# Two-phase fp32 kernel on one core: new order of the seven-product sums, an earlier split of w_out2, and GpSimd for the operands' low parts

## What is computed

```python
# attention part, batch 8, 8 heads, S = 576, head size 64
kv  = einsum('bhsd,bhse->bhde', k, v)
out = einsum('bhsd,bhde->bhse', q, kv)
x   = out / sqrt(mean(out**2) + 1e-6) * g_norm          # -> (8, 576, 512)
# first MLP
h = relu(x @ w_in); u, v = h[..., :512], h[..., 512:]
v_n = (v - mean(v)) / sqrt(var(v) + 1e-6)
x = (u * (w_spatial @ v_n + b_spatial)) @ w_out
# second MLP
h = relu(x @ w_in2)                                      # 512 -> 1024
conv = 3-tap convolution of h along S, one set of taps per feature
out = (h * sigmoid(conv)) @ w_out2                       # 1024 -> 512
```

## Time and profile before

| | us |
|---|---|
| median of 3 runs | 841.52 (839.79 to 842.79) |
| the profiled execution's own time | 841.8 |
| its span, first to last instruction | 840.0 |
| PE busy | 802.4 (96%) |
| DVE busy | 607.5 (72%) |
| ACT busy | 418.3 (50%) |
| POOL busy | 41.1 (5%) |

### The profile page before, as it was taken

One profiled execution on the slowest core, in us unless ns is written; L12 is line 12 of the kernel. 1 busy time (PEld: TensorE's weight loads), 2 busy tenths in 40 slices (PEclk: granted clock), 3 DMA queues, 4 the chain that ended last, 5 costly groups with the idle time before them and its releaser, 6 DMA issues.

```text
span 840.0 us, 16008 instructions
## 1 busy us (share of the span) xinstructions
PE 802.4 (96%) x5910; PEld 704.0 (84%) x5910; DVE 607.5 (72%) x1254; ACT 418.3 (50%) x753; POOL 41.1 (5%) x44
## 2 busy tenths in 40 slices
PE   8998999999999999999969999999999999999998
PEld 7678899897979899898868897978879797796976
DVE  3876666757665766758869878597885978669782
ACT  4654352526343443524715648456473655646563
POOL 3342000000000000000140000000000000000000
PEclk9999999999999999999979999999999999999999
DMA  9862433426262533331322111121201212102101
GB/s 317 276 238 58 181 115 120 179 75 248 71 253 57 197 105 116 106 92 64 114 85 99 51 35 65 64 99 51 99 22 42 98 50 98 50 13 98 50 1 62
DMA packets 34009, 88.48 MB, mean 105 GB/s; under 512 B 2514, under 2 KB 8882, under 8 KB 30004
## 3 DMA queue, kind: packets, MB, share of 16 engines
q1 hardware_dynamic: 33828, 87.99, 31.0%
q10 hardware_dynamic: 144, 0.01, 0.0%
HBM read 61.92 MB, written 26.08 MB: 105 GB/s over the span
## 4 chain that ended last, share of the span: by engine, by line
PE 71%; DVE 18%; ACT 4%; issue 4%; DMA 2%; SPq 0%; DVEq 0%; ACTq 0%
PE ps L446 23%; PE ps L622 17%; PE ps L614 14%; PE ps L477 11%; DVE h_and_sums L1172 3%; DVE work L1213 3%; DVE work L1208 3%; PE ps L397 2%; DVE v_hg_split L1219 2%; PE ps L413 2%; ACT v_hg_split L897 2%; DMA kv_raw<-kv_rest_dram 1%; PE ps L547 1%; DVE t_then_s L1092 1%; PE ps L425 1%
## 5 line engine op out<-in xcount | busy, mean ns | idle before, releaser
L622 PE MATMUL ps<-w_in_split,v_hg_split 128*128 128x512 f32 x832 | 209.1, 398 | 14.7 <-DVE v_hg_split L1219 13.9
L622 PEld LDWEIGHTS ps<-w_in_split,v_hg_split 128*128 128x128 f32 x832 | 151.8, 188 | 66.0 <-DVE v_hg_split L1219 33.5
L446 PE MATMUL ps<-w_sp_split,v_hg_split 128*128 128x288 f32 x896 | 122.2, 297 | 2.8 <-DVE w_sp_split L1061 2.4
L446 PEld LDWEIGHTS ps<-w_sp_split,v_hg_split 128*128 128x128 f32 x896 | 120.8, 190 | 3.5 <-issue 2.6
L446 PE MATMUL ps<-x_operand_split,w_in_split 128*128 128x288 f32 x768 | 104.3, 296 | 1.5 <-ACT work L704 1.5
L446 PEld LDWEIGHTS ps<-x_operand_split,w_in_split 128*128 128x128 f32 x768 | 102.2, 188 | 3.6 <-ACT work L704 1.9
L477 PE MATMUL ps<-w_in_split,x_operand_split 128*128 128x512 f32 x384 | 93.5, 396 | 0.0
L477 PEld LDWEIGHTS ps<-w_in_split,x_operand_split 128*128 128x128 f32 x384 | 70.4, 188 | 20.9 <-issue 6.1
L1172 DVE TENSOR_TENSOR h_and_sums<-t_then_s,ps 128x288 f32<-128x288 f32 x64 | 28.0, 453 | 62.0 <-PE ps L614 41.5
L1172 DVE TENSOR_TENSOR h_and_sums<-h_and_sums,ps 128x288 f32<-128x288 f32 x160 | 66.2, 449 | 8.2 <-PE ps L614 7.4
L614 PE MATMUL ps<-x_operand_split,w_combined_more 128*128 128x288 f32 x384 | 62.3, 298 | 0.0
(11 more groups left out here) (124 smaller groups left out, 1137.4 us busy)
## 6 DMA issues: line engine op xcount, KB each, us to landing
kv_raw<-kv_main_dram SPq DMA_DIRECT2D x8, 2048.0 KB, 9.7
q_raw<-q_T_dram SPq DMA_DIRECT2D x8, 1152.0 KB, 5.3
operand_scratch<-t_then_s SPq DMA_DIRECT2D x8, 1152.0 KB, 5.3
operand_raw<-operand_scratch SPq DMA_DIRECT2D x8, 1152.0 KB, 5.5
out_dram<-work SPq DMA_DIRECT2D x32, 256.0 KB, 2.2
sq_then_r<-r_scratch SPq DMA_DIRECT2D x14, 576.0 KB, 6.3
operand_scratch<-work SPq DMA_DIRECT2D x24, 288.0 KB, 2.6
operand_more_raw<-operand_scratch SPq DMA_DIRECT2D x8, 864.0 KB, 7.2
```

Source lines behind the costliest of these rows:

```text
L446: last = pe.matmul(pair[bank][:, c, :], st, mo[:, c * HALF:(c + 1) * HALF], start=(n == 0), stop=(n == len(steps) - 1))
L622: last = pe.matmul(PS[:, ROW_BANK[i], :], x, wout2[:, w, F_ORDER[e], :], start=(e == 0 and n == 0), stop=(e == FT - 1 and n == len(PASSES) ...
```

## The change

1. The seven products come in the order A11, S2, A12, S1, S4, S3, A22, and the sums of a group follow in the order u2, C11, u4, C12, u3, C22, C21 (before: u2, C11, u3, u4, C22, C21, C12). The upper feature block of a group is complete after sum 4, the lower after sum 7, and `F_ORDER` takes them in turn.
2. The queues of `body2` on ACT and DVE are written out by hand instead of by a loop over e. `h_lo(0)` and `h_lo(1)` stand within the sums of groups 2 and 3.
3. For the batches ahead, `operand_lo` moves from DVE to POOL, and ACT makes three of the seven high parts ahead of its last two `h_hi`.
4. w_out2 is loaded in two halves by DMAs in ACT's queue in batches 1 and 2 of the first phase, split there by ACT (four instructions a batch) and POOL, sent to a scratch in HBM (2 MB each half), and loaded back split (four DMAs, 4.2 MB in all) ahead of the second phase.
5. `square_sum` contracts all 128 partitions: 16 matmuls for 32 before, and the inverse root works on 144 columns for 288.
6. For the last batch the T blocks are made within the sums of the second phase's first group. The waits on the stores move from the head of the second phase to the first `sigmoid` and the first copy out. A12 and A22 get other places for their high parts, with one wait less.

The core of the diff:

```diff
-PRODUCTS = [(A11, B11), (S2, T2), (A12, B21), (S3, T3), (S1, T1), (A22, T4), (S4, B22)]
+PRODUCTS = [(A11, B11), (S2, T2), (A12, B21), (S1, T1), (S4, B22), (S3, T3), (A22, T4)]
-LAST_SUM = [None, 0, 1, 2, 4, 5, 6]
-F_ORDER = [4, 0, 5, 1, 6, 2, 7, 3]
-TOP_SUM, LOW_SUM = 6, 5
+LAST_SUM = [None, 1, 2, 6, 4, 5, 7]
+F_ORDER = [0, 4, 1, 5, 2, 6, 3, 7]
+TOP_SUM, LOW_SUM = 4, 7
...
+            def operand_lo(b, k):
+                o = PRODUCTS[k][1]
+                pool.wait_ge(s_ophi, b * NPROD + k + 1)
+                pool.tensor_tensor(operand[o][:, LO, :], operand_raw[o], operand[o][:, HI, :].bitcast(F32),
+                                   ALU.subtract).then_inc(s_oplo, 1)
...
+                    if isinstance(b, int) and b in (1, 2):
+                        if i == 0:
+                            wo2_load(b - 1)
+                        else:
+                            wo2_split(b - 1, i - 1)
...
+            def wo2_split(h, f):
+                act.wait_ge(s_wo2_in, (h + 1) * DMA)
+                act.activation(wo2_hi[:, f, :], wo2_raw[:, f, :], ACT.Copy).then_inc(s_wo2_hi, 1)
...
-                for e in range(FT + 2):
-                    if e < FT:
-                        h_relu(b, e)
-                        tap1(b, e)
-                    if e >= 2:
-                        h_hi(b, odd, e - 2)
-                    if 0 <= e - 1 < FT:
-                        sigmoid(b, e - 1)
-                    if e + 1 < GROUPS:
-                        first_copy(b, e + 1)
+                h_relu(b, 1)
+                first_copy(b, 1)
+                tap1(b, 1)
+                sigmoid(b, 0)
+                h_relu(b, 2)
+                sigmoid(b, 1)
+
+                tap1(b, 2)
+                first_copy(b, 2)
+                h_hi(b, odd, 0)
+                h_relu(b, 3)
+                tap1(b, 3)
+                sigmoid(b, 2)
+                h_relu(b, 4)
+
+                first_copy(b, 3)
...
+                h_hi(b, odd, 5)
+                sigmoid(b, 7)
+                if ahead:
+                    operand_hi(b + 1, 0)
+                    operand_hi(b + 1, 1)
+                h_hi(b, odd, 6)
+                if ahead:
+                    operand_hi(b + 1, 2)
+                h_hi(b, odd, 7)
```

More of the change, by code:

```diff
@@ L151, in build @@
         u2, u3, u4 = (HB[:, o + i * HALF:o + (i + 1) * HALF] for i in range(3))
[L152 to L155, removed]
+        t_sb = [WK[:, 0:S], WK[:, 3840:3840 + S]]
+        x1 = [WK[:, S:S + HALF], WK[:, 3328:3328 + HALF]]
+        p_sb = [WK[:, 1024 + i * S:1024 + (i + 1) * S] for i in (0, 1)]
         def gated(k, l):
@@ L1221, in body2 @@
             def body2(b, odd, ahead):
-                sums_a(b, 0)
-                sums_b(b, 0)
-                sums_c(b, 0)
-                for e in range(FT + 2):
-                    g = e + 1
-                    if g < GROUPS:
-                        sums_a(b, g)
-                    if e < FT:
-                        tap0(b, e)
-                    if g < GROUPS:
-                        sums_b(b, g)
-                    if e >= 2:
-                        h_lo(b, odd, e - 2)
-                    if e < FT:
-                        tap2(b, e)
-                    if g < GROUPS:
-                        sums_c(b, g)
-                    if 0 <= e - 1 < FT:
-                        mul(b, e - 1)
@@ L1241, in body2 @@
-                if ahead:
-                    for k in range(NPROD):
-                        operand_lo(b + 1, k)
+                first = isinstance(b, int) and b == 0
+                sum_u2_c11(b, 0)
+                if first:
+                    t_a(B - 1)
+                sum_u4(b, 0)
+                sum_c12(b, 0)
+                if first:
+                    t_b(B - 1)
+                sum_u3(b, 0)
+                if first:
+                    t_c(B - 1)
+                sum_c22(b, 0)
@@ new lines, in body2 @@
+                sum_c21(b, 0)
+                sum_u2_c11(b, 1)
+                tap0(b, 0)
+                sum_u4(b, 1)
+                tap2(b, 0)
+                sum_c12(b, 1)
+                sum_u3(b, 1)
+                tap0(b, 1)
+                sum_c22(b, 1)
+                sum_c21(b, 1)
+                tap2(b, 1)
+                sum_u2_c11(b, 2)
+                mul(b, 0)
+                sum_u4(b, 2)
+                tap0(b, 2)
+                sum_c12(b, 2)
+                sum_u3(b, 2)
@@ new lines, in body2 @@
+                h_lo(b, odd, 0)
+                sum_c22(b, 2)
+                sum_c21(b, 2)
+                tap2(b, 2)
+                sum_u2_c11(b, 3)
+                mul(b, 1)
+                sum_u4(b, 3)
+                tap0(b, 3)
+                sum_c12(b, 3)
+                sum_u3(b, 3)
+                h_lo(b, odd, 1)
+                sum_c22(b, 3)
+                sum_c21(b, 3)
+                tap2(b, 3)
+                mul(b, 2)
+                for e in range(4, FT):
+                    tap0(b, e)
+                    h_lo(b, odd, e - 2)
+                    tap2(b, e)
+                    mul(b, e - 1)
@@ L1245, in _ @@
+                h_lo(b, odd, FT - 2)
+                mul(b, FT - 1)
+                h_lo(b, odd, FT - 1)
             for i in range(FT):
```

196 lines of the change are left out of this document (124 added, 72 removed).

## The result

| | before | after |
|---|---|---|
| median, us | 841.39 (839.79 to 842.79) | 874.88 (872.61 to 875.95) |
| span of the profiled execution | 840.0 | 872.1 |
| second phase begins | 416.84 | 433.11 |
| batches 0, 1, 2, 3 of the second phase | 60.82, 53.70, 47.74, 53.82 | 52.93, 57.12, 52.24, 57.29 |
| mean granted TensorE clock | 0.992 | 0.982 |

The change makes the kernel slower: ratio 1.0395, 95% interval 1.0365 to 1.0425. The direction was forecast, the size was not: +33.5 us where +15.3 was forecast, and 874.9 lies above the range. The 32.1 us of span fall into two halves of like size: 16.3 in the first phase (forecast +6.4), 15.8 in the second (forecast +8.9). Of the 16.3, 2.4 us are a start-up that came later in this execution, which differs from run to run.

A forecast was written before the change was run, and what follows sets the result against it. It took second-phase row steps to be bound by the ACT-DVE chain, 2.98 us against the PE's 2.73. Terms 6.4 - 8.0 + 16.9 = +15.3 gave 856.8 us; range 838 to 863 for 8 in 10.

The forecast's parts named there:

- beside the other I take 6 (bounds 4 and 8): First phase, batches 1 and 2: w_out2's load beside the kv load lands in 6 us; +3.2 us a batch.
- The sum: Whole kernel: first phase +6.4, second phase's batch 0 -8.0, its batches 1 to 7 +16.9, together +15.3 us.
- the forecast wait on the squares: First phase, batches 1 and 2: fourth square starts at 18.5 instead of 15.6, so the PE waits 1.3 us.
- the exclusion: Second phase, batch end: DVE and POOL lock each other out of one port pair; even batch 50.5, without it 49.25.
- The walk: Each engine's fixed queue followed forward with traced durations; gave +2.9 us for an even second-phase batch, +2.6 for an odd one.
- The price from the earlier trace: DVE subtractions beside POOL take 1.77 us against 0.75 alone; DVE waits 1.25 us for a 576-column POOL instruction.
- a lag of 2.4: Second phase, batch 0: T blocks and pad memsets put DVE's seventh sum 2.4 us late, a lag that stays.
- the tail: Second phase, batch end: early high parts and POOL delay the last `h_lo` to 47.7 us from 44.4; batch ends at 50.5.
- The openings of groups 2 and 3: Second phase: ACT's opening copies stand behind sigmoids, so DVE idles about 1.9 us per group.
- Rival 2: Second phase: group openings not late, `h_lo(2)` done at 27.9 us, row steps closed but for the tail; 823 us, chance 0.15.
- Rival 1: Second phase: POOL barely hinders DVE; even batches 49.25, odd 55.15 us, total 846 us, chance 0.17.
- rival 3: Gains and losses cancel: load lands in 4 us, `square_sum` gains 4, POOL costs half; 842.5 us, chance 0.10.

The follow-up runs named there:

- the larger pieces: Changed kernel with w_out2's rows dealt so each partition reads one 8 KB piece instead of four of 2 KB (output of permuted rows): 866.85 us.
- C and D undone: Changed kernel with all seven high parts back behind the last `h_hi` and the low parts back on DVE: 848.32 us.
- the three ways of A: Changed kernel with w_out2's splits behind u's relus, or its load one batch earlier, or its load in 8 KB pieces: 855.51, 856.62, 866.85 us.
- B: Changed kernel with the first copies of groups 2 and 3 moved ahead of the sigmoids in ACT's queue: 846.01 us.
- A, B and C with D: Changed kernel with w_out2's splits behind u's relus, first copies early, high parts late, low parts on DVE; all together: 803.00 us.

## Why the prediction was wrong

**The step that failed first: "beside the other I take 6 (bounds 4 and 8)".** The load of w_out2 landed in 14.2 and 10.1 us. The sum had the kv load running from 2.5 us into the batch. SP's timelines have it issued at 5.0 before the change (238.44, the batch begins at 233.40) and at 5.1 in batch 1 after it, and the q load at 13.6 in both. So kv was still on its way when w_out2's load was issued, 8.3 us in, and q, which the sum left out, came before it had landed. Issued ahead of the others it does land in 6.5 us (load one batch earlier): 6 was the price of another place in the program. A better upper bound is an estimate from all bytes in flight: kv's 2304 KB, q's 1152 and the load's 1024 are 4.6 MB, at the 331 GB/s of the window after the change 13.9 us. That it comes so near to 14.2 is in part luck: some of kv had been moved by 100.20, and a store of 1152 KB issued at 95.99 was still on its way.

**What the wait costs a second time.** Neither PE wait was forecast above 2 us, and the clock not at all; the forecast wait on the squares did not come. In a batch without a wait, the matmuls of the rest and the sum of squares take 3.0 us from the start of one to the end of the other (219.34 to 222.36). Behind the wait of 7.32 us in batch 1 they take 5.5, behind the 3.15 us of batch 2 5.9, and with the larger pieces 5.5 behind 3.83 us and 4.7 behind 2.54. So the lower clock cost 2.5, 2.9, 2.5 and 1.7 us there: much the same behind 3.2 us as behind 7.3. In all, batches 1 and 2 cost 10.6 + 6.5 = 17.1 where 6.4 was taken: 10.5 of waiting, 5.4 of clock, and the rest for the splits and what follows from them (0.6 a batch in the load-early kernel).

**What the first phase gave back** was missed: its batch 0 takes 49.4 us for 52.1. The sum said that the PE doesn't wait for DVE in the first phase, which is true of steady batches only: in batch 0 the PE's wait for the spatial weights' low parts fell from 2.41 us to 1.27, and the spatial products behind it take 15.08 us for 16.61 (15.01 in a steady batch). In the profile of after this is hidden by the start-up that came 2.4 us later (the second kv product starts at 38.8 to 42.5 us in the profiles here). The row of before:

```profile
75.66 16.61 PE L446 MATMUL ps<-w_sp_split,v_hg_split 128*128 128x288 f32 x112 [2.41 <-DVE w_sp_split L1061]
```

That the shorter inverse root is what frees it was not tried by itself. `square_sum` takes 1.19 us for 1.24: worth nothing, as taken.

**POOL beside DVE: right mechanism, a term too small.** The sum gave the exclusion 1.25 us in an even batch (50.5 against 49.25) and 1.2 in an odd one. Undoing it gave 2.9 and 2.1. The walk took `h_lo(6)` as one instruction that waits once. It is two, and POOL slips an instruction in between: `h_lo(6)` is done 45.1 us into the batch where 43.8 was forecast (POOL began at 41.76, forecast 41.75), `mul(7)` starts behind a third one, and `h_lo(7)` is done at 48.5 for 47.7. That is 0.8 of the 1.7 us by which an even batch is late (52.24 for 50.5). The other 0.9 us are the clock once more, which was at 0.52 for 3.5 us behind the 2.39 us wait. The price from the earlier trace rows was right: 1.90 less 0.68 and 1.96 less 0.75 are 1.2 us lost by each of these two instructions. The Trainium skill ("SBUF — State Buffer", section "SBUF: two separate sides") has the loser of the port pair blocked for the whole instruction of the other; the runs agree, with 1.2 us of POOL's 1.5 as the part that DVE sees.

**Right by luck.** Batch 0 of the second phase took 52.93 us for the 52.9 of the sum, an even batch of 50.5 and a lag of 2.4. The even batch takes 52.24, and with C and D undone batch 0 is only 1.6 us longer than batch 2: the tail was taken too small and the lag too large. The clock also stayed at 1.00 in its last two steps; in the three kernels with an unchanged second phase (the three ways of A) it fell behind the same wait, and batch 0 took 53.7 to 53.8.

**Right, and to how much.** The openings of groups 2 and 3: idle 1.80 and 1.71, released by ACT's copy. `sigmoid(7)` and two high parts put `h_hi(6)` at 585.32, 42.2 into the batch, as forecast. The PE waited ahead of step 6, as forecast, but ahead of step 7 only 0.5 us or less, not over 1. The stores and the loads of w_out2's halves ahead of the second phase cost nothing. Rival 2 failed where it was said to be decided: the openings were late, and step 2, which needs `h_lo(2)`, starts at 30.8 us (30.7 forecast, 27.9 by the rival). Undo just that (B) and the row steps run closed up to the tail; undo the tail too and the gain is larger than the rival had it. Rival 1's batches came out within 0.02 us once POOL was taken away. Of rival 3 neither the load in 4 us nor a gain in `square_sum` came.

**How the parts add up.** In even batches undoing C and D takes 52.2 to 48.2, and undoing B as well to 44.8, 3.4 less and 2.9 below the old 47.74. Alone, B takes off 3.3 to 4.2, so opening and tail overlap by less than 1 us. Undone one at a time, A, B and C with D bring 19.4, 28.9 and 26.6 us, 74.9 in all; together they bring 71.9. The fourth part, the low parts on POOL, costs 6.7 us even where nothing else is in its way.

## What to carry to other kernels

Price a load by everything that is in flight beside it, and put what waits for it where nothing that the PE needs stands behind it in the queue: the same load, landing no earlier, cost 17 us of the first phase in one place and nothing in another. In a handwritten queue, ask of each copy that opens the next stage whether the instruction ahead of it waits for the last one of this stage; undoing two such copies brought more here than undoing any other single part. Work given to an idle engine is not free when it shares a port with the busy one: count how many instructions of each alternate, and whether the slower engine still delivers by the time of use.

## What the runs showed of the hardware

- A DVE instruction with both inputs in SBUF lost 1.2 us beside POOL instructions of about 1.5 us (`h_lo`'s main part 1.90 us for 0.68, `mul` 1.96 for 0.75). The first part of `h_lo`, which met only the end of a POOL instruction, took 0.40 us for 0.23.
- Behind PE waits of 7.3, 3.8, 3.2 and 2.5 us in the first phase, the rows at the lower clock took 2.5, 2.5, 2.9 and 1.7 us more. Behind a wait of 2.4 us in batch 0 of the second phase the clock fell in three kernels (7.1 to 7.2 us for two steps) and stayed at 1.00 in the changed one (6.3 us).
- A load of 1 MB on ACT's queue, beside kv and q loads on SP's, landed in 14.2 and 10.1 us in 528 packets of 2 KB, and in 10.7 and 9.5 in 144 packets (7.3 KB on average). Issued 10 us ahead of them it landed in 6.5 and 5.8.
